# One word per expert block, a loop in two halves, row copies on VectorE and the last wait on SyncE

## What is computed

```python
state = gamma[None, :, None, None] * state + np.einsum('bhd,bhe->bhde', k[:, :, t], v[:, :, t])
y[:, :, t] = scale * np.einsum('bhd,bhde->bhe', q[:, :, t], state)
...
logits = x @ w_gate + modality_bias[modality_id]
e_idx = np.argmax(logits, axis=1)
...
for e in range(E):
    mask = e_idx == e
    h = np.maximum(x[mask] @ w1[e], 0.0)
    out[mask] = gate_w[mask, None] * (h @ w2[e])
...
a = x @ w1
b = x @ w2
h = a * b @ w3
return (h @ w_out).astype(np.float32)
```

## Time and profile before

| | us |
|---|---|
| median of 3 runs | 849.05 (848.98 to 850.65) |
| the profiled execution | 853.0 |
| its span, first to last instruction | 851.1 |
| PE busy | 823.1 (97%) |
| PE weight loads busy | 705.3 |
| DVE busy | 414.7 |
| ACT busy | 292.4 |
| POOL busy | 176.5 |
| mean granted TensorE clock | 0.988 of full |

### The profile page before, as it was taken

The page is one execution under the profiler, slowest core; times in us unless marked ns, Lnnn a source line. Parts: engine busy times, 40 slices in busy tenths (PEclk is TensorE's granted clock), DMA queues, the critical chain, the costliest instruction groups (busy, mean ns, idle before and its releaser), DMA issues.

```text
span 851.1 us, 14864 instructions
## 1 busy us (share of the span) xinstructions
PE 823.1 (97%) x5578; PEld 705.3 (83%) x5579; DVE 414.7 (49%) x662; ACT 292.4 (34%) x467; POOL 176.5 (21%) x207
## 2 busy tenths in 40 slices
PE   9899999998999999999998899999999999999995
PEld 8899878787999998888886678888888888888884
DVE  3667788630213144111142887762577742778400
ACT  1234423331222244212143545522545423454210
POOL 2223002202020120201001334311433311433011
PEclk9999999999999999999999899999999999999999
DMA  9999992423030343210231211141112231111010
GB/s 324 326 316 314 290 352 94 149 100 101 0 100 0 99 148 116 81 49 20 79 114 59 62 52 50 50 149 50 51 51 73 81 106 49 63 50 50 12 50 37
DMA packets 51456, 91.88 MB, mean 108 GB/s; under 512 B 8529, under 2 KB 15313, under 8 KB 51409
## 3 DMA queue, kind: packets, MB, share of 16 engines
q1 hardware_dynamic: 41728, 68.47, 24.0%
q0 software_dynamic: 4736, 14.72, 5.2%
q10 hardware_dynamic: 4946, 8.08, 2.8%
HBM read 71.03 MB, written 20.22 MB: 107 GB/s over the span
## 4 chain that ended last, share of the span: by engine, by line
PE 89%; DVE 6%; issue 2%; ACT 1%; ACTq 1%; DVEq 0%; POOL 0%
PE bank L444 35%; PE attn L444 32%; PE pair L444 8%; PE bank L970 3%; PE attn L997 3%; PE pair L982 3%; PE pair L1075 2%; PE bank L1009 1%; PE attn L988 1%; PE bank L947 1%; PE bank L1158 1%; ACTq L393 1%; DVE wlo L1255 0%; DVE w3T L1255 0%; PE pair L954 0%
## 5 line engine op out<-in xcount | busy, mean ns | idle before, releaser
L444 PE MATMUL bank<-xT,we_p 128*128 128x512 f32 (+1 forms) x672 | 141.9, 372 | 4.9 <-issue 3.6
L444 PEld LDWEIGHTS bank<-xT,we_p 128*128 128x128 f32 x672 | 124.5, 192 | 21.9 <-issue 6.0
L444 PE MATMUL attn<-hT,we_p 128*128 128x512 f32 (+1 forms) x672 | 141.8, 368 | 0.0
L444 PEld LDWEIGHTS attn<-hT,we_p 128*128 128x128 f32 x672 | 121.3, 188 | 14.4
L444 PE MATMUL attn<-wc,gT 128*128 128x512 f32 x576 | 132.5, 390 | 0.2
L444 PEld LDWEIGHTS attn<-wc,gT 128*128 128x128 f32 x576 | 107.9, 188 | 23.8 <-DVE gT L1255 1.5
L1501 DVE SCALAR_TENSOR_TENSOR hT<-bank,hT 128x512 fp32r<-128x512 f32 x56 | 38.7, 691 | 152.7 <-ACT hT L741 152.7
L444 PE MATMUL bank<-yhi,whi 128*128 128x512 f32 x240 | 94.6, 394 | 3.4 <-issue 3.4
L444 PE MATMUL bank<-yhi,wlo 128*128 128x512 f32 x240 | 94.1, 392 | 0.0
L741 ACT ACTIVATE hT<-bank 128x512 fp32r<-128x512 f32 x56 | 33.5, 599 | 104.3 <-PE bank L444 104.3
L635 POOL TENSOR_TENSOR w_raw<-a,w_raw 128x256 f32<-128x256 f32 x24 | 23.9, 994 | 184.1 <-DMA w_raw<-in_moe_w_dram 184.1
(11 more groups left out here) (198 smaller groups left out, 1218.6 us busy)
## 6 DMA issues: line engine op xcount, KB each, us to landing
we_raw<-in_moe_w_dram SPq DMA_DIRECT2D x6, 2048.0 KB, 9.4
w_raw<-in_moe_w_dram SPq DMA_DIRECT2D x40, 256.0 KB, 2.7
yT_sorted<-yout ACTq DMA_DIRECT2D x7, 1024.0 KB, 4.8
qkv<-in_q_t_dram SPq DMA_DIRECT2D x24, 256.0 KB, 3.4
qkv<-in_v_dram SPq DMA_DIRECT2D x24, 256.0 KB, 5.1
x_rows<-x_keep SPq DMA_DIRECT2D x24, 256.0 KB, 3.5
qkv<-in_k_t_dram SPq DMA_DIRECT2D x23, 256.0 KB, 5.0
qkv<-in_k_dram SPq DMA_DIRECT2D x20, 256.0 KB, 5.2
```

Of the source, the lines that this page charges most:

```text
L444: i = pe.matmul(out_, left(a), right(b), start=(first and n == 0), stop=(last and n == 2), **kw)
```

## The change

It joins these edits:

- `each_window` walks two halves of HW = 8 laps. A half is entered only if it has a block, and the block number is the sum of half and lap.
- `win_tab` has three columns: first row, first tile, and a word with size + 8 x flag + 16 x run. TensorE, ScalarE and VectorE load the word once a block and take it apart with masks and shifts; the flag of the next block is read by one load of the next word.
- One-tile block: the copies to `h_rows` are made by VectorE, interleaved with its w2 pieces; the branch on the flag is around the whole hidden part, so copies and relus stand in it twice. Semaphore counts are adapted.
- `dve.sem_inc(s_hlo, 2)` stands before the last two `wc_lo`, and TensorE's wait on `s_wclo` before its loop is gone.
- The wait on the scatters' landing is SyncE's last instruction instead of GpSimd's.

```diff
@@ -66,8 +66,9 @@
...
     MINW = NT // GT
+    HW = 8
     WARM = 10
-    assert H * D == DM and DM == BANK and 2 * D == P and GT == B and FF == 2 * BANK and KF == 2 * B and NI % 2 == 1 and NG % 2 == 0 and KD == 4
+    assert H * D == DM and DM == BANK and 2 * D == P and GT == B and FF == 2 * BANK and KF == 2 * B and NI % 2 == 1 and GT < 8 and E <= 8 and NW <= 2 * HW and NG % 2 == 0 and KD == 4
@@ -137,7 +138,7 @@
...
         win_meta = fixed("win_meta", [P, GT, 2])
-        win_tab = fixed("win_tab", [1, NW + 1, 5], I32)
+        win_tab = fixed("win_tab", [1, 2 * HW + 1, 3], I32)
         need_tab = fixed("need_tab", [1, NG], I32)
@@ -382,9 +383,12 @@
...
             total = eng.value_load(num_tab[0:1, 1:2], min_val=MINW, max_val=NW)
-            with eng.Fori(0, NW) as w:
-                with eng.If(total > w):
-                    body(w, total)
+            with eng.Fori(0, 2) as half:
+                with eng.If(total > half * HW):
+                    with eng.Fori(0, HW) as i:
+                        w = eng.snap(half * HW + i)
+                        with eng.If(total > w):
+                            body(w, total)
             return total
@@ -392,16 +396,28 @@
...
-        NEW_RUN, RUN_OF, START, SIZE, TILE = range(5)
-
-        def is_new(eng, w):
-
-            return table(eng, w, NEW_RUN, 0, 1)
-
-        def if_new(eng, new, w, body):
-
-            with eng.If(new > 0):
-                body(table(eng, w, RUN_OF, 0, E - 1))
+        START, TILE, WORD = range(3)
+
+        def word_of(eng, w):
+
+            return table(eng, w, WORD, 1, 16 * E - 1)
+
+        def size_in(word):
+
+            return word & 7
+
+        def new_in(word):
+
+            return (word >> 3) & 1
+
+        def run_in(eng, word):
+
+            return eng.snap(word >> 4)
+
+        def if_new(eng, word, body):
+
+            with eng.If(new_in(word) > 0):
+                body(run_in(eng, word))
@@ -571,6 +587,8 @@
...
                     w_load(n)
+            for i in range(2):
+                sp.wait_ge(s_out[i], 16 * NT // 2)
@@ -653,9 +671,6 @@
...
                                             otile[:, n % 2, :], None).then_inc(s_out[n % 2], 16)
-            for i in range(2):
-                pool.wait_ge(s_out[i], 16 * NT // 2)
-
@@ -791,10 +806,8 @@
...
                         h_hi(w, f)
-                        if f == 0:
-                            this = is_new(act, w)
                         if f in (1, 3):
-                            if_new(act, this, w, lambda run: w2_hi(run, range(f - 1, f + 1)))
+                            if_new(act, word, lambda run: w2_hi(run, range(f - 1, f + 1)))
@@ -818,16 +831,20 @@
...
                 def one_tile_hidden():
-                    this = is_new(act, w)
-                    if_new(act, this, w, lambda run: w2_hi(run, range(0, 2)))
-                    for half in range(2):
-                        act.wait_ge(s_hp, w * KF + (half + 1))
-                        copy(h_rows[:, half * BANK:(half + 1) * BANK], bank[half][:, :]).then_inc(s_hhi, 1)
-                    for half in range(2):
+                    def relu(half):
                         act.wait_ge(s_hp, w * KF + (half + 1) * (GT - 1) + 2)
                         act.activation(hT[:, HI, half * GT:(half + 1) * GT, 0:P], bank[half][:, :].rearrange("p (f t) -> p f t", f=GT),
-                                       ACT.Relu).then_inc(s_hhi, GT - 1)
-                    if_new(act, this, w, lambda run: w2_hi(run, range(2, 4)))
+                                       ACT.Relu).then_inc(s_hhi, GT)
+
+                    with act.If(new_in(word) > 0):
+                        run = run_in(act, word)
+                        w2_hi(run, range(0, 2))
+                        relu(0)
+                        relu(1)
+                        w2_hi(run, range(2, 4))
+                    with act.If(new_in(word) < 1):
+                        relu(0)
+                        relu(1)
@@ -848,13 +865,13 @@
...
-                size = table(act, w, SIZE, 1, GT)
+                word = word_of(act, w)
+                size = size_in(word)
                 with act.If(size > 1):
...
                     one_tile_hidden()
-                coming = is_new(act, w + 1)
-                if_new(act, coming, w + 1, w1_hi)
+                if_new(act, word_of(act, w + 1), w1_hi)
                 with act.If(total < w + 2):
@@ -1098,7 +1115,6 @@
...
                 def wide(tiles):
-                    run = table(pe, w, RUN_OF, 0, E - 1)
                     n = tiles * P
@@ -1119,14 +1134,14 @@
...
                     for half in range(2):
-                        pe.wait_ge(s_hhi, w * KF + (half + 1))
+                        pe.wait_ge(s_hlo, w * KF + (half + 3))
                         for t in range(GT):
...
                         if f % GT == 0:
-                            pe.wait_ge(s_hlo, w * KF + (f + GT + 2))
+                            pe.wait_ge(s_hlo, w * KF + (GT + (f // GT + 1) * (GT - 1)))
                         if f % 2 == 0:
@@ -1138,7 +1153,8 @@
...
-                size = table(pe, w, SIZE, 1, GT)
+                word = word_of(pe, w)
+                size, run = size_in(word), run_in(pe, word)
                 with pe.If(size > 3):
@@ -1164,7 +1180,6 @@
...
             pe.wait_ge(s_tab, 1)
-            pe.wait_ge(s_wclo, KF - 2)
             each_window(pe, window)
@@ -1459,12 +1474,12 @@
...
             link(ts(w_k[:, 2, :], w_k[:, 2, :], e_sc[one, LAST, 0:1], None, ALU.min))
-            col = lambda a, c: win_tab[:, a:, c:c + 1].rearrange("p a b -> p (a b)")
-            link(ts(win_tab[:, 0:1, NEW_RUN:NEW_RUN + 1].rearrange("p a b -> p (a b)"), w_k[:, 2, 0:1], 0.0, 1.0, ALU.mult, ALU.add))
-            link(tt(col(1, NEW_RUN), w_k[:, 2, 1:], w_k[:, 2, 0:n_tab - 1], ALU.subtract))
-            link(dve.tensor_copy(col(0, RUN_OF), w_k[:, 2, :]))
+            col = lambda a, c: win_tab[:, a:n_tab, c:c + 1].rearrange("p a b -> p (a b)")
+            link(ts(w_k[:, 4, 0:1], w_k[:, 2, 0:1], 0.0, 1.0, ALU.mult, ALU.add))
+            link(tt(w_k[:, 4, 1:], w_k[:, 2, 1:], w_k[:, 2, 0:n_tab - 1], ALU.subtract))
+            link(dve.scalar_tensor_tensor(w_k[:, 4, :], w_k[:, 4, :], 8.0, w_k[:, 0, :], ALU.mult, ALU.add))
+            link(dve.scalar_tensor_tensor(col(0, WORD), w_k[:, 2, :], 16.0, w_k[:, 4, :], ALU.mult, ALU.add))
             link(dve.tensor_copy(col(0, START), w_k[:, 1, :]))
-            link(dve.tensor_copy(col(0, SIZE), w_k[:, 0, :]))
             link(dve.tensor_copy(col(0, TILE), w_k[:, 5, :]))
@@ -1485,6 +1500,7 @@
...
             w1_lo(0, early_chunks(5))
+            dve.sem_inc(s_hlo, 2)
             wc_lo(6)
@@ -1551,34 +1567,47 @@
...
                         h_lo(w, f)
-                        if f == 0:
-                            this = is_new(dve, w)
                         if f in (1, 3):
-                            if_new(dve, this, w, lambda run: w2_lo(run, range(f - 1, f + 1)))
+                            if_new(dve, word, lambda run: w2_lo(run, range(f - 1, f + 1)))
                 def one_tile_hidden():
-                    this = is_new(dve, w)
-                    if_new(dve, this, w, lambda run: w2_lo(run, range(0, 2)))
-                    for half in range(2):
-                        dve.wait_ge(s_hhi, w * KF + (half + 1) * (GT - 1) + 2)
+                    def rows_copy(half):
+                        dve.wait_ge(s_hp, w * KF + (half + 1))
+                        dve.tensor_copy(h_rows[:, half * BANK:(half + 1) * BANK], bank[half][:, :]).then_inc(s_hlo, 1)
+
+                    def relu_lo(half):
+                        dve.wait_ge(s_hhi, w * KF + (half + 1) * GT)
                         fs = slice(half * GT, (half + 1) * GT)
                         dve.scalar_tensor_tensor(hT[:, LO, fs, 0:P], bank[half][:, :].rearrange("p (f t) -> p f t", f=GT), 0.0,
-                                                 hT[:, HI, fs, 0:P].bitcast(F32), ALU.max, ALU.subtract).then_inc(s_hlo, GT)
-                    if_new(dve, this, w, lambda run: w2_lo(run, range(2, 4)))
-
-                size = table(dve, w, SIZE, 1, GT)
+                                                 hT[:, HI, fs, 0:P].bitcast(F32), ALU.max, ALU.subtract).then_inc(s_hlo, GT - 1)
+
+                    with dve.If(new_in(word) > 0):
+                        run = run_in(dve, word)
+                        rows_copy(0)
+                        w2_lo(run, (0,))
+                        rows_copy(1)
+                        relu_lo(0)
+                        w2_lo(run, (1,))
+                        relu_lo(1)
+                        w2_lo(run, (2, 3))
+                    with dve.If(new_in(word) < 1):
+                        rows_copy(0)
+                        rows_copy(1)
+                        relu_lo(0)
+                        relu_lo(1)
+
+                word = word_of(dve, w)
+                size = size_in(word)
                 with dve.If(size > 1):
...
```

(6 more changed lines are left out.)

## The result

| | time, us | ratio to before, 95% interval |
|---|---|---|
| before, in the same comparison | 849.85 (848.98 to 851.96, 4 runs) | |
| changed | 840.02 (838.76 to 844.0, 4 runs) | 0.9886 [0.9863, 0.991] |
| changed, profiled execution | 839.66, span 837.9, granted clock 0.992 | |
| forecast | 842.6 (839.0 to 846.0) | |

The change took 9.8 us off, where 6.5 were forecast. A second set of four runs (840.61, first experiment, 8.6 us under the runs of before beside it) makes the median of all eight 840.4. The two profiled executions lie further apart, 853.0 and 839.66, since that of before lies high among its runs. Of those 13.3 us some 3 lie ahead of the stop at the first block, where no edit touches TensorE's work (block 0 begins at 160.50 and at 156.56, of which 0.93 was that stop).

A forecast was written before the change was run, and what follows sets the result against it. TensorE was taken to bound the kernel (89% of the last-ending chain). 0.9 + 1.0 - 0.3 + 3.1 + 1.8 = 6.5 us off the 849.05 median gave 842.6 us, range 839.0 to 846.0.

The forecast's parts named there:

- Start of block 0: TensorE's first block: issuing VectorE's starting increment two wc pieces earlier removes a wait, gaining 0.9 us.
- From block 0 to block 1: TensorE's 3.40 us stop there: one table load fewer, less added register operations, shortens it by 1.0 us.
- The lower value, 0.45: Gain in us before block 1 if the remaining TensorE table load took the slow 882 ns.
- The other block changes: Two changes between three-tile blocks, paced by ScalarE: added sum and mask lose 0.3 us, bounds 0 and 0.6.
- code was not fetched again: Slower rival: bigger ScalarE and VectorE bodies no longer stay loaded, stops at block changes cost 18.8 us, 861.4; chance 0.04.
- The one-tile block and the last stage: Last block's earlier copies and w2, plus fewer empty laps, start the last stage 3.1 us sooner, bounds 1.9 and 3.9.
- The tail: End of kernel: with SyncE waiting, GpSimd's DRAIN starts beside the scatter's landing, gaining 1.8 us, bounds 0 and 1.85.
- My sign for "wrong", a DRAIN of 7 us: Kernel's end: a GpSimd DRAIN of 7 us instead of 5.3 was to show the forecast wrong.
- The clock: Rival: the shorter stop before block 1 keeps TensorE's clock up, saving 3.0 us more, 839.6; chance 0.22.
- Laps, nine blocks: Rival: second half entered, three laps more, last stage gains about 1.5 less, 844.1; chance 0.20 shared with other rivals.
- drain waits: Rival: GpSimd's DRAIN waits for the scatter's data, tail gives nothing, 844.4; chance 0.20 shared with other rivals.

The follow-up runs named there:

- first experiment: The changed kernel measured again with no edit, as base for the other runs on that chip: 840.61 us, 0.9887 of the kernel before.
- the word alone: The kernel before with only the packed word in a three-column table; loop, start, row copies and last wait as before: 844.94 us, 0.9945.
- the halves alone: The kernel before with only the two-half loop and the longer table: 847.09 us, 0.9978.
- tail: The changed kernel with the wait on the scatters' landing put back from SyncE to GpSimd: 842.46 us, 0.9913.
- start late: The changed kernel with VectorE's starting increment back behind all wc pieces and TensorE's wait on six wc pieces back: 841.26 us, 0.9909.
- one load: The changed kernel with one unused table load added to TensorE's queue at the end of block 0, behind a branch: 843.35 us, 0.9927.
- two loads: The changed kernel with two unused table loads added to TensorE's queue at the end of block 0, behind a branch: 845.31 us, 0.9953.
- split: The changed kernel with the last outward column of a four-tile block moved behind the branches for the other sizes: 841.98 us, 0.991.
- the split kernel before: The kernel before with only the last outward column of a four-tile block moved behind the branches for sizes: 849.9 us, 1.0009.
- flat loop: The changed kernel with one loop of 13 laps again instead of two halves: 840.72 us, 0.9898.
- the one-tile block as before: The changed kernel with row copies back on ScalarE behind two w2 pieces, keeping the one word load: 840.91 us, 0.9886.
- order: The changed kernel with VectorE's lower part for the last stage's second factor made ahead of the fourth sum: 840.91 us, 0.9892.

## Why the prediction was right, and where it was not

**Start of block 0** (0.9): right, 0.98 us back in the trace when undone.

**From block 0 to block 1** (1.0): right in kind, 1.4 in size (3.40 to 2.00). The load that is left took 319 ns and not 882, as I chose, and the long jump was 0.22 us shorter, which is chance: it took 3.59 to 4.17 us in the profiles with the word, and the stop 1.96 to 2.54. The lower value, 0.45, was not the case.

**The other block changes** (0.3 lost): from 35.74 and 35.73 us to 36.00 and 36.00, 0.5 lost. Between the two three-tile blocks' ScalarE store and its first relu lie 2.83 us for 2.72, so that this gives 0.1 of the 0.26 each; the rest I can't place. It comes with the word and not with the halves: the word alone has 36.00 and 36.01, the halves alone 35.82 and 35.71. The blocks of four tiles behind them show nothing (45.35, 45.31, 45.31 in both). So code was not fetched again: from 240 to 488 us after has one instruction transfer, of 0.01 MB, and before has one from 248 to 498. The Trainium skill ("Runtime: NRT & Kernel Launch", Instruction fetch mechanics) says that a taken branch to outside the two pages at hand has to fetch its target first. This case's traces agree for the first pass of the long jump, with its transfer of instructions, and not for the later ones: the seven others of L1160 took 0.07 to 0.24 us, and a second loop edge cost nothing that can be seen (stops before block 1 of 3.45 and 3.40 us with and without it).

**The one-tile block and the last stage** (3.1): 3.06 in the profile of after, and right in nearly each time there. Behind the block's first matmul:

| | forecast | after |
|---|---|---|
| w2 starts on ScalarE | 4.16 | 4.03 |
| outward product starts | 7.8 | 7.60 |
| outward product ends | 13.6 | 13.68 |
| first sum on VectorE | 12.0 | 12.03 |
| factor 2 of the last stage | 21.9 | 21.98 |
| b_sum ends, VectorE's side | 32.8 | 32.62 |
| third factor | 33.6 | 33.69 |

The new wait for the lower part (5.1 forecast, 4.62), the drop of the clock behind it and TensorE as the last to come all stood in the working. That the last line fits to 0.1 us is luck in part: the forecast has 2.2 us lost to the clock, and this profile has a spell of 6.8 us. Of seven profiles with this same last stage (after, repeated, tail, start late, one load, two loads, split) five have a spell of 3.4 us and the third factor at 32.88 to 33.28, and two have 6.8 and 33.69 and 34.32. The median is 33.10, a gain of 3.65 on the 36.75 of before (the split kernel before has 37.25). The stretch of after that answers to the earlier trace rows:

```profile
469.10:473.40 4.30, 4.29 (x10) 3.42 (x11) 4.30 (x5) 2.39 (x4) 0.02 (x1) 0.50 0.00 0
```

What the working didn't see is whose gain it is. I gave 2.0 us to the copies and loads and 2.0 to the laps, as a sum of 4.0 on VectorE's side. They are substitutes: the word alone gives 3.05, the halves alone 1.3, and with the word in place neither the halves (0.3 by the median, none by the segment) nor the copies (none) give more. That holds with like clocks compared: with 6.8 us of the lower level the word alone has 33.70 and after 33.69; with 3.4 us the flat loop has 32.86, the one-tile block as before 32.68 and the full change 32.88 to 33.28, but the halves alone 35.41.

Why the word suffices can be read from factor 2, which needs two things, factor 1 on TensorE behind its laps and the lower part from VectorE:

| | factor 1 starts | lower part ends | factor 2 starts |
|---|---|---|---|
| before | 21.90 | 23.92 | 24.59 |
| halves alone | 18.00 | 24.08 | 24.13 |
| word alone | 19.39 | 21.27 | 22.09 |
| flat loop | 18.57 | 21.44 | 21.49 |
| after | 15.73 | 21.93 | 21.98 |

In before TensorE comes to factor 2 only 0.7 us behind the lower part. The halves speed up only factor 1, so that factor 2 then waits for the lower part. The word alone moves factor 1 by 2.5 us and the lower part by 2.7. With it the laps lie where TensorE would otherwise wait for the lower part: with them factor 2 starts at 22.09 and 21.49, without them at 21.98.

**The tail** (1.8): right, 1.95, and for the reason given (the last scatter of before ends at 843.65, by the earlier trace rows, where the working had 843.75). My sign for "wrong", a DRAIN of 7 us, nearly appeared (6507 ns) though nothing was wrong: the record starts before the scatter is issued. The end of the record should have been named, not its length.

**The clock** (rival, 0.22; 839.6): this is the term that was mis-sized. The places of the sum give 0.9 + 1.4 - 0.5 + 3.06 + 1.95 = 6.8 us, the medians 8.6 to 9.8. The mean granted clock of the runs was 0.9856 in 18 runs of before and 0.993 in the four of the repeated change. 0.0074 of 850 us is 12.6 us at the lower level less, and so up to 6.3 us of time, if TensorE had work in all of it. Two places show it. Block 1 took 38.28 us in before and 36.93 in the halves alone, which has the same stop; with a stop of 2.0 to 2.5 us it was 35.14 in three profiles (after, start late, flat loop) and 36.7 in five (repeated, tail, one-tile, order, word alone). So the rival, which gave back all of the 3.0 us, was right in three cases of eight, and in the other five the spell was 3.4 us. The forecast left the clock where it was, at 3.0 us lost behind that stop; on average about 1.5 came back (37.6 against 36.1). The other place is the last stage, with 0.6 us more than the 3.06 of the one profile. An estimate from these profiles is then 6.8 + 1.5 + 0.6 = 8.9 us, within what the medians say; with so few profiles of before it can be off by one. The range held because it took this rival in.

**Laps, nine blocks** and **drain waits**: neither was the case. Eight gathers ran again, and the DRAIN ended 5.31 us behind the scatter's end with the scatter still landing.

## What to carry to other kernels

Where an engine's queue is not ahead of its work, count the instructions that the page calls not busy: one table load of 0.3 to 0.9 us, a register operation, a lap are then time of the kernel, and packing fields into one word pays there; between the three-tile blocks it cost 0.26 us each time. Gains that feed one and the same waiting instruction can be substitutes, so test each edit alone on the old kernel and taken out of the new one before giving any of them its share. And a shorter stop of TensorE can give back more than its length, since the clock behind it may stay up, as it did in three profiles of eight here.

## What the runs showed of the hardware

- **The drain.** GpSimd's DRAIN at the end lasts 5.31 us from the moment its last instruction is done, with nothing outstanding (5306 ns in the five profiles where GpSimd waits for the scatters first) and with a scatter still landing (5.31). So the landing of the scatter can lie beside it, as here.
- **The clock after a stop.** With a stop of 1.96 to 2.54 us on the same place the clock fell to the lower level for 3.4 us in five of eight profiles and not at all in three. With 3.40 and 3.45 us it was 6.8 and 3.4; with 4.96 and 5.72, 6.8 in both. Behind the wait of 4.0 to 4.6 us in the last stage of the changed kernel it was 3.4 in five profiles and 6.8 in two. One profile can't say what a stop costs.
- **The first long jump.** 3.5 to 4.2 us the first time, in twelve profiles, and a median of 0.15 over the passes; 5.2 and 5.5 with one small branch more; and a second fetch behind it, with a stop of TensorE of 2.7 and 3.0 us beside it in the two runs that put work there.
